# Fused attention and two MLPs: the bias tables of pairs 2 and 3 are made between the normalisations, and v and four w_in tiles are loaded ahead of pair 2

## What is computed

```python
q, k, v: (4, 8, 576, 64)            # batch, heads, sequence, head size
scores = scale * q @ k.T
mask = (rel >= 0) & (rel < 128)     # rel = query position - key position
scores = where(mask, scores - slope[h] * abs(rel), -1e9)
attn = softmax(scores); x = attn @ v            # as 2304 tokens of 512
h = max(x @ w_in, 0);   x2 = (h * h) @ w_out    # 512 -> 2048 -> 512
h = x2 @ w_in2;         out = (h * cos(h)) @ w_out2
```

## Time and profile before

| | us |
|---|---|
| median of 3 runs (911.34 to 912.75) | 912.34 |
| the profiled execution | 912.75 |
| its span, first to last instruction | 910.6 |
| TensorE busy | 894.9 (98%) |
| VectorE busy | 518.6 (57%) |
| ScalarE busy | 369.2 (41%) |
| GpSimd busy | 193.7 (21%) |

### The profile page before, as it was taken

How to read it: one execution, slowest core, us unless ns; L and a number is a source line. 1 busy time by engine, 2 the same in 40 slices (tenths; PEclk the granted TensorE clock), 3 DMA queues, 4 the chain that set the end, 5 groups by cost and what they waited for, 6 DMA issues and landing times.

```text
span 910.6 us, 17307 instructions
## 1 busy us (share of the span) xinstructions
PE 894.9 (98%) x6128; PEld 840.7 (92%) x6128; DVE 518.6 (57%) x1239; ACT 369.2 (41%) x886; POOL 193.7 (21%) x298
## 2 busy tenths in 40 slices
PE   6999899999999999999999999999999999999998
PEld 4888799999999999999999989999999899999987
DVE  6888553333333332332353878777676776777675
ACT  7888232223232222222232344444444443443433
POOL 9888992000000000000069910000000000000000
PEclk9999999999999999999999999999999999999999
DMA  7776520000000000000134200100100100100101
GB/s 245 251 248 199 165 70 1 1 0 0 0 0 0 0 0 0 0 0 0 46 117 128 80 2 1 35 0 0 35 0 0 35 0 0 35 0 0 35 1 35
DMA packets 22922, 40.15 MB, mean 44 GB/s; under 512 B 3680, under 2 KB 8800, under 8 KB 22880
## 3 DMA queue, kind: packets, MB, share of 16 engines
q1 hardware_dynamic: 22016, 38.77, 13.1%
q10 hardware_dynamic: 864, 0.82, 0.3%
HBM read 34.87 MB, written 4.72 MB: 43 GB/s over the span
## 4 chain that ended last, share of the span: by engine, by line
PE 95%; DVE 2%; POOL 2%; issue 1%; ACT 0%; DVEq 0%; ACTq 0%; POOLq 0%
PE psum L497 43%; PE psum L531 22%; PE psum L516 21%; PE psum L458 4%; PE psum L416 3%; PE psum L370 2%; POOL probs L319 1%; PE psum L379 0%; DVE g_lo L773 0%; DVE work L811 0%; DVE pt L750 0%; POOL win_lo L325 0%; DVE work L804 0%; DVE work L814 0%; POOL bias L309 0%
## 5 line engine op out<-in xcount | busy, mean ns | idle before, releaser
L497 PE MATMUL psum<-xs,win_hi 128*128 (+1 forms) x1536 | 391.6, 335 | 0.0
L497 PEld LDWEIGHTS psum<-xs,win_hi 128*128 128x128 f32 x1536 | 279.4, 188 | 8.4
L497 PE MATMUL psum<-xs,win_lo 128*128 (+1 forms) x768 | 257.8, 336 | 0.0
L602 ACT ACTIVATE g_hi<-work 128x384 fp32r<-128x384 f32 x192 | 101.0, 526 | 218.6 <-DVE work L790 153.9
L773 DVE TENSOR_TENSOR g_lo<-work,g_hi 128x384 fp32r<-128x384 f32 x192 | 119.2, 621 | 57.4 <-ACT g_hi L602 57.4
L780 DVE SCALAR_TENSOR_TENSOR work<-psum,work 128x384 f32<-128x384 f32 x96 | 53.4, 557 | 170.6 <-ACT work L607 170.3
L497 PEld LDWEIGHTS psum<-xs,win_lo 128*128 128x128 f32 x768 | 144.1, 188 | 0.0
L531 PE MATMUL psum<-g_hi,wout_hi 128*128 128x384 f32 x384 | 128.3, 334 | 0.0
L531 PE MATMUL psum<-g_lo,wout_hi 128*128 128x384 f32 x384 | 128.3, 334 | 0.0
L531 PE MATMUL psum<-g_hi,wout_lo 128*128 128x384 f32 x384 | 128.3, 334 | 0.0
L607 ACT ACTIVATE work<-psum 128x384 f32<-128x384 f32 x96 | 47.1, 491 | 193.2 <-PE psum L497 193.2
(11 more groups left out here) (60 smaller groups left out, 955.5 us busy)
## 6 DMA issues: line engine op xcount, KB each, us to landing
win_raw<-w_in SPq DMA_DIRECT2D x32, 256.0 KB, 3.3
v_raw<-v SPq DMA_DIRECT2D x16, 512.0 KB, 3.2
wout_raw<-w_out SPq DMA_DIRECT2D x32, 256.0 KB, 3.3
q_raw<-q_t SPq DMA_DIRECT2D x15, 288.0 KB, 3.5
k_raw<-k_t SPq DMA_DIRECT2D x15, 288.0 KB, 4.7
out<-x SPq DMA_DIRECT2D x10, 192.0 KB, 1.9
out<-x SPq DMA_DIRECT2D x12, 128.0 KB, 1.7
out<-x SPq DMA_DIRECT2D x10, 64.0 KB, 1.6
```

The lines of the kernel that those rows point to most:

```text
L497: last = pe.matmul(o, wi[:, f, w], xs[:, bass.ds(par, 1), part, k, :], start=(k == 0 and n == 0), stop=(k == DT - 1 and n == 2))
L602: act.activation(g_hi[:, f % HID_RING, :], work2[:, f % 2, :], ACT.Copy).then_inc(g_hi_ready, 1)
```

## The change

SP's order in the first microseconds changes. The first w_in tile goes ahead of q and k of pair 1, the second behind them; v of pairs 0 and 1 and two further w_in tiles follow before q and k of pair 2. In before, v of pair 0 and 1 stood behind q and k of pairs 2 and 3. EARLY_WIN is 4 in place of 2, so the later w_in tiles are each issued two steps sooner.

GpSimd makes only table set 1 ahead of the first weight splits. Set 2 is made after normalise(0) and set 3 after normalise(1). The waits on distance_ready, upper_ready and slopes_ready move into the function.

```diff
-EARLY_WIN = 2
+EARLY_WIN = 4
...
             sp.dma_start(q_raw[:, 0, 0:FIRST], q_t[0, :, 0:FIRST]).then_inc(qk_landed[0], 16)
+            load_win(0)
             load_qk(1)
-            for f in range(EARLY_WIN):
+            load_win(1)
+            load_v(0)
+            load_v(1)
+            for f in range(2, EARLY_WIN):
                 load_win(f)
             for p in range(PAIRS + 1):
                 if p + 2 < PAIRS:
                     load_qk(p + 2)
-                if p < V_RING:
-                    load_v(p)
-                elif p > V_RING:
+                if p > V_RING:
                     load_v(p - 1)
...
             def bias_tables(d):
+                if d == 1:
+                    pool.wait_ge(distance_ready, 3)
+                    pool.wait_ge(upper_ready, 1)
+                    pool.wait_ge(slopes_ready, 1)
                 for h in (2 * d, 2 * d + 1):
...
-            pool.wait_ge(distance_ready, 3)
-            pool.wait_ge(upper_ready, 1)
-            pool.wait_ge(slopes_ready, 1)
-            for d in range(1, H // 2):
-                bias_tables(d)
             order = 0
...
             for s in range(PAIRS + 1):
                 if s >= 1:
                     normalise(s - 1)
+                if s < H // 2 - 1:
+                    bias_tables(s + 1)
                 while order < min(ATTENTION_WIN, 2 + 2 * s // 3):
```

## The result

| | median us | runs |
|---|---|---|
| before | 912.2 | 4 |
| changed kernel | 917.74 (916.9 to 919.36) | 4 |
| ratio | 1.0063 (95% interval 1.0046 to 1.0082) | |

The changed kernel is slower by 5.5 us, 0.63%. The forecast was slower by 3.2 us (915.5, range 914.5 to 917.5): the sign was right and both new waits came where they were forecast, but the size was too small and the time lies just outside the range. The profiled execution of the changed kernel took 917.79 us, near its median; that of before, at 912.75, lay 0.55 above its median. So of the 5.5 us the two profiles can show 5.0.

A forecast was written before the change was run, and what follows sets the result against it. The fill was taken as bound by ScalarE's exponentials, TensorE without slack from values(0) to 90 us. Late tables move values(0) from 21.74 to 24.92, 3.18 us: 912.75 gives 915.9, against the median 912.34 gives 915.5; range 914.5 to 917.5.

The forecast's parts named there:

- the mark: Start of values(0), TensorE's first product with values: forecast to move from 21.74 to 24.92 us, 3.18 later.
- the wait at 16.81: TensorE's 1.67 us idle before five transposes; forecast held it ended by ScalarE's copy at 16.66, not by GpSimd.
- the first hole: VectorE waits for table 2 before pair 2's first pass, 16.47 in place of 12.08 us: 4.39 us.
- the second hole: VectorE waits for table 3, ready at 23.40, before pair 3's first pass at 23.50 us; 2 to 3 us idle.
- the late landing of pair 2's load: Pair 2's k, behind more loads, lands near 14.6 in place of 10.9 us; mostly hidden, taken as 0.
- a standing VectorE speaks for 1.57: GpSimd's late table sets: 1.57 us each taken, since VectorE stands still; at 1.98 each, 0.82 us more.
- the clock term: TensorE's low clock: hidden if ahead of 24.92 us, 1.5 us if behind; the latter rival 917.0, chance 0.14.
- The inverse of pair 0 at 11.18: VectorE's reciprocal, from 10.96 for 0.22 us, ends at 11.18; normalise(0) on GpSimd then starts at 11.28.
- the rival's price of 4.7: Same two VectorE waits, low clock behind values(0)'s start: 3.18 + 1.52 = 4.70 us, 917.0, chance 0.14.
- VectorE was not served early: Rival: GpSimd's 18 normalisations and two tables run far faster, so VectorE has no hole: 910.8 us, chance 0.03.
- set 3 was not early enough: Rival: table 3 early enough, TensorE at full clock, only VectorE's first wait counts: +1.4 us, 913.8, chance 0.07.
- the queue of loads: Rival: loads run at 235 GB/s, pair 2 lands at 18.6 us and becomes the bound: 6.0 us, 918.3, chance 0.06.

The follow-up runs named there:

- e14: The kernel before, no edit, one more profiled execution: span 910.2 us, pair 4's scores at 24.39 us.
- e2: The kernel before with its own loads, table sets 2 and 3 late as in the changed kernel: 917.74 us, ratio 1.0063.
- e10: The kernel before with its own loads, only table set 3 made behind normalise(1): 914.78 us, ratio 1.0023.
- e8: The changed kernel with only set 2 behind its normalisation, set 3 made in front: 914.76 us, ratio 1.0037.
- e15: The changed kernel, no edit, one more profiled execution: span 914.2 us, pair 4's scores at 28.14 us.
- e16: The kernel before, no edit, one more profiled execution: span 909.2 us, pair 4's scores at 23.02 us.
- e13: The changed kernel, no edit, one more profiled execution: span 916.3 us, pair 4's scores at 30.50 us.
- e4: The kernel before with 12 unread identity transposes in TensorE's idle time ahead of 16.81 us: 911.36 us, ratio 0.9991.
- e12: The changed kernel with six products of zeros at the start and 26, 22 and 17 transposes in TensorE's three gaps: 917.47 us, ratio 1.0053.
- e7: The changed kernel with table sets 2 and 3 each ahead of the normalisation in place of behind it: 914.38 us, ratio 1.0025.
- e11: The kernel before with six products of zeros at the start and 12 transposes in TensorE's idle time ahead of 16.81: 910.75 us, ratio 0.9981.
- e5: The kernel before with ten products of zeros at the start and 12 transposes in TensorE's idle time ahead of 16.81: 912.36 us, ratio 1.0002.
- e1: The changed kernel's new loads alone, all three table sets in front as before: 914.35 us, ratio 1.0022.
- e3: The changed kernel with 17 unread identity transposes in TensorE's idle time ahead of values(0): 917.92 us, ratio 1.0062.
- e9: The kernel before with its own loads, only table set 2 made behind normalise(0): 917.14 us, ratio 1.0048.

## Why the prediction missed

**Right.** That TensorE is fed from the mark on and the shift is carried unchanged to the end; that ScalarE's copy, not GpSimd, ended the wait at 16.81 (e14, the same kernel as before, names it in its own row, below); the first hole with its size (4.24 for 4.39) and its chain; the second hole (2.99) and that values(0) waits for pair 3's passes; the late landing of pair 2's load (13.8 for 14.6), hidden by the first hole in the profile (and e2, without the new loads, takes as long); no cost of pair 1's load. TensorE in e14, with the ScalarE copy as releaser of the same five transposes:

```profile
16.55 0.74 PE L416 MATMUL psum<-ident,probs 128*128 128x128 f32 x5 [1.47 <-ACT pt L588]
```

**Too small, 0.5 us: the mark itself.** It came at 25.42 for 24.92. Set 3 took 21.84 to 23.79, 1.95 us, where the sum had 1.57, and GpSimd began it 0.08 after its normalisations. The other 0.04 is pair 3's five passes and the last handoff (0.14 more than worked out) less the steps that came early (0.10). The upper bound of 1.98 had been kept. The step that failed is that a standing VectorE speaks for 1.57: it stood still here, and set 2 took 1.6 and set 3 1.95. In e10, 20.17 to 22.13 is again 1.96. The slow set is set 3 wherever it stands, in the earlier trace rows too, and in e8, where set 3 is made second, at 4.6 us, it takes 1.96 there and set 2, made last, 1.6; so neither the place nor VectorE's work beside it is the cause. The instructions of set 3 last no longer; they start further apart. The first two starts of set 2 and of set 3 in the changed kernel:

```profile
14.76 0.35 POOL L315 TENSOR_SCALAR bias<-distance 128x192 f32<-128x192 f32 x1
15.08 0.30 POOL L316 TENSOR_SCALAR bias_first<-distance 128x128 f32<-128x128 f32 x1
...
21.84 0.35 POOL L315 TENSOR_SCALAR bias<-distance 128x192 f32<-128x192 f32 x1
22.25 0.30 POOL L316 TENSOR_SCALAR bias_first<-distance 128x128 f32<-128x128 f32 x1
```

It is 0.32 us from start to start in set 2 and 0.41 in set 3. What spreads them is open.

**Wrong, 1.5 us: the clock term.** "A low stretch ahead of 24.92 is hidden by the wait for table 3. One that falls behind it costs 1.5 us in full", with a chance of 0.14 for the second. In two of the three profiled executions of the changed kernel the stretch fell behind the mark. The sum compared a mark of before that carried 1.52 us of half clock with a mark of the changed kernel that carried none; e15 against e16 shows what the holes cost on equal terms, 5.1 us. By the steps: 3.18 and 0.50 for the mark, and 4.36 - 2.86 = 1.50 behind it make the 5.18 at pair 4.

In place of that term the runs show about 5.1 us for the two holes like against like, and single executions from 28.14 to 30.50 at pair 4 according to where half clock falls. How the executions behind the median are divided among these kinds is open: only three executions of the changed kernel have a trace.

**A step taken as fixed, which costs both kernels.** The inverse of pair 0 at 11.18 was taken as fixed. It hangs on TensorE's scores of pair 1, and in executions that run those at half pace it comes 0.9 later (12.04 in e13); the mark of the changed kernel then moves by as much (26.30 for 25.42). It is no part of the miss, for before has it too: in e4's profiled execution the inverse of pair 0 came at 12.34, ScalarE's copy ended at 17.62, 1.0 later than in e16, and values(0) started at 21.70 in place of 20.12, some 0.7 of that from the 12 transposes of the filling, which ran on past the copy:

```profile
17.05 0.57 ACT L591 ACTIVATE pt<-psum 128x512 f32<-128x512 f32 x1
...
17.06 1.47 PE L559 MATMUL psum<-ident 128*128 128x128 f32 x12
18.37 0.71 PE L416 MATMUL psum<-ident,probs 128*128 128x128 f32 x5
```

So the rival's price of 4.7 was right for one kind of execution, the two holes with a stretch behind the mark, but for the slow set 3; its chance was too small.

The other rivals fell: VectorE was not served early, set 3 was not early enough, and the queue of loads did not bind in the profile, though in e12 its late load outlasted the first hole.

## What to carry to other kernels

When work is moved from the front of an engine's queue into its gaps, put it ahead of the step whose input is late, not behind it: the same two table sets cost 3.3 us less one place earlier (e7 against the change). Before one execution's mark is compared with a sum, ask whether it holds a stretch at half clock, and charge the same to both sides; otherwise the sum subtracts a loss that the new kernel will have too. Idle TensorE in a fill can be filled with products that nobody reads: here 1.7 us for a kernel that was otherwise left as it was (e11). Too many of them put off the work behind them (e5, e4 and e12), and in the changed kernel, whose path to the mark runs over GpSimd and VectorE, filling gained nothing that the medians show.

## What the runs showed of the hardware

- The granted clock in the records is 1.00 from the start in every execution, also while TensorE runs at half pace: 32 score products take 2.62 us at 4 us where 1.42 is usual, and in e2 the 24 at 8.75 take 1.98 for 1.10 with the record still at 1.00. Here only stretches after the first recorded change could be read from it; before that the durations tell.
- How long this first slow stretch lasts differs between executions of one kernel: pair 1's scores are at full pace in before, after, e1, e7, e8, e14, e15 and e16, and at half pace in e2, e3, e4, e9, e10 and e13. With six products of zeros ahead (e11) the scores of pair 1 ran at full pace.
- The five instructions of table set 3 take 1.95 to 2.0 us, those of sets 1 and 2 1.56 to 1.61, in every place tried; single instructions last as long in all three (0.35 and 0.30 us for the first two), but start up to 0.1 us further apart in set 3.
